# Eight sums of x per tile made by VectorE in place of GpSimd, in a three-layer float32 kernel on one Trainium2 core

## The reference

```python
def _moe_ref(x, w_in, w_out):
    h = x @ w_in                                  # 3072x512 by 512x2048
    g = np.where(h > 0.0, h, np.exp(np.minimum(h, 0.0)) - 1.0)
    return g @ w_out                              # 2048x512

def _moe2_ref(x, w_in, w_out, s, b):
    r = np.maximum(x @ w_in, 0.0)
    return (s * (r * r) + b) @ w_out
```

## Time and profile before

| | us |
|---|---|
| median of 3 runs | 1146.09 |
| lowest, highest | 1142.92, 1147.23 |
| the profiled execution | 1145.91 |
| its span in the profile | 1143.90 |
| PE busy | 1098.1 |
| DVE busy | 822.1 |
| ACT busy | 781.3 |
| POOL busy | 389.7 |

### The profile page before, as it was taken

The page is one execution under the profiler, slowest core; times in us unless marked ns, Lnnn a source line. Parts: engine busy times, 40 slices in busy tenths (PEclk is TensorE's granted clock), DMA queues, the critical chain, the costliest instruction groups (busy, mean ns, idle before and its releaser), DMA issues.

```text
span 1143.9 us, 18152 instructions
## 1 busy us (share of the span) xinstructions
PE 1098.1 (96%) x5787; PEld 876.1 (77%) x5787; DVE 822.1 (72%) x1210; ACT 781.3 (68%) x1842; POOL 389.7 (34%) x427
## 2 busy tenths in 40 slices
PE   8999898979999999989999999999999999999998
PEld 4667666757767778878788787888888888888886
DVE  5796686458886965898877968868848568576475
ACT  4797686667658757758758678667677476774574
POOL 5789689741232432136276113663000000000000
PEclk9999999989999999999999999999999999999999
DMA  9998999989889989869899789898697666776664
GB/s 202 268 273 254 345 330 354 348 268 323 251 237 251 269 256 263 280 210 348 301 358 348 233 263 373 300 349 282 186 282 233 189 198 189 219 218 193 194 192 158
DMA packets 204054, 302.80 MB, mean 265 GB/s; under 512 B 112824, under 2 KB 121016, under 8 KB 203960
## 3 DMA queue, kind: packets, MB, share of 16 engines
q1 hardware_dynamic: 203960, 301.65, 85.4%
HBM read 226.10 MB, written 75.50 MB: 264 GB/s over the span
## 4 chain that ended last, share of the span: by engine, by line
PE 73%; ACT 6%; DMA 6%; DVE 5%; issue 4%; POOL 3%; SPq 3%; ACTq 0%; POOLq 0%; DVEq 0%
PE ps L1020 35%; PE ps L1005 31%; DMA w_scratch<-w_new 3%; ACT ps L1100 2%; PE ps L914 2%; DMA w_ring<-w_scratch 1%; DVE g_lo L1494 1%; PE ps L939 1%; POOL w_new L801 1%; PE ps L966 1%; POOL att L801 1%; ACT elu L1193 1%; PE ps L923 1%; PE ps L908 1%; DVE nbias L1347 1%
## 5 line engine op out<-in xcount | busy, mean ns | idle before, releaser
L1005 PE MATMUL ps<-xc_hi,w_ring 128*128 128x512 f32 x1344 | 435.9, 397 | 5.0 <-ACT s L1166 3.7
L1020 PE MATMUL ps<-g_hi,w_ring 128*128 128x512 f32 x1344 | 420.4, 394 | 11.4 <-issue 6.4
L1005 PEld LDWEIGHTS ps<-xc_hi,w_ring 128*128 128x128 f32 x1344 | 253.9, 189 | 63.8 <-issue 4.0
L1020 PEld LDWEIGHTS ps<-g_hi,w_ring 128*128 128x128 f32 x1344 | 249.9, 189 | 68.3 <-issue 9.0
L1005 PE MATMUL ps<-xc_lo,w_ring 128*128 128x512 f32 x672 | 263.2, 392 | 0.0
L1020 PE MATMUL ps<-g_lo,w_ring 128*128 128x512 f32 x672 | 263.1, 392 | 0.0
L801 POOL TENSOR_TENSOR w_new<-w_raw,w_new 128x256 fp32r<-128x256 f32 x179 | 165.9, 933 | 219.0 <-ACT w_new L1247 215.8
L1494 DVE TENSOR_TENSOR g_lo<-X,g_hi 128x512 fp32r<-128x512 f32 x240 | 178.4, 748 | 30.5 <-ACT g_hi L1233 30.0
L1233 ACT ACTIVATE g_hi<-X 128x512 fp32r<-128x512 f32 x240 | 150.1, 629 | 56.8 <-PE ps L1020 55.1
L1020 PEld LDWEIGHTS ps<-g_lo,w_ring 128*128 128x128 f32 x672 | 126.7, 189 | 26.9
L1005 PEld LDWEIGHTS ps<-xc_lo,w_ring 128*128 128x128 f32 x672 | 127.2, 189 | 24.4
(11 more groups left out here) (125 smaller groups left out, 1350.5 us busy)
## 6 DMA issues: line engine op xcount, KB each, us to landing
w_ring<-w_scratch SPq DMA_DIRECT2D x336, 512.0 KB, 4.4
w_scratch<-w_new SPq DMA_DIRECT2D x179, 256.0 KB, 5.3
w_scratch<-att SPq DMA_DIRECT2D x45, 256.0 KB, 4.8
w_raw<-in_moe_w_in SPq DMA_DIRECT2D x16, 512.0 KB, 5.6
w_raw<-in_moe_w_out SPq DMA_DIRECT2D x16, 512.0 KB, 6.0
x_scratch<-y SPq DMA_DIRECT2D x12, 512.0 KB, 6.1
att<-x_scratch SPq DMA_DIRECT2D x12, 512.0 KB, 5.9
out<-elu SPq DMA_DIRECT2D x24, 256.0 KB, 4.3
```

The source lines that it names most:

```text
L1005: last = nc.tensor.matmul(bank_of(st, st.i), w[:, a, cols], x[:, st.pi, kk, :], start=(st.pi in (P1, P5) and kk == 0 and n == 0), stop=(kk ...
L1020: last = nc.tensor.matmul(bank_of(st, d), w[:, a, cols], x[:, k % RING, :], start=(st.pi in (P1, P5) + (P4,) * (1 - st.gr) and st.i == 0 a ...
```

## The change

POOL's `sums_of_x` and its two calls go. DVE gets `next_x_sum`, called in each step at the end of its list (before the copy of K^T), for the steps in the table `NEXT_SUMS`: P5 at 106 and 107, P6 at 108 and 109, P7 at 110 and 111, P4 at 114 and 115, each first kk = 0 and then kk = 1. Operands, results and shapes are unchanged; the count in `x_sum` follows the new order. The P4 sums lie in the next tile's steps 2 and 3.

```diff
+NEXT_SUMS = {106 + i: (pi, kk) for i, (pi, kk) in enumerate((pi, kk) for pi in (P5, P6, P7) for kk in range(2))}
+NEXT_SUMS.update({114: (P4, 0), 115: (P4, 1)})
...
         def x_sum(t, kk, pi):
             first = HEAD_SUMS + 8 * (t - 1)
-            return first + (7 + kk if pi == P4 else 3 * kk + {P5: 1, P6: 2, P7: 3}[pi])
+            return first + 2 * (P5, P6, P7, P4).index(pi) + kk + 1
...
-            def sums_of_x(t):
-                n = HEAD_SUMS + 8 * (t - 1)
-                for kk in range(2):
-                    pool.wait_ge(x_in[kk], 32 * t)
-                    x12, x22 = (x_from(t, kk, pi) for pi in (P7, P3))
-                    x11 = x_from(t, kk, P1)
-                    t2 = x_from(t, kk, P6)
-                    pool.wait_ge(x_lo_done, x_count(t) + x_index(t, kk, P1) + 1)
-                    nc.gpsimd.tensor_tensor(x11, x12, x11, ALU.subtract).then_inc(x_sums, 1)
-                    pool.wait_ge(x_sums, n + 3 * kk + 1)
-                    nc.gpsimd.tensor_tensor(t2, x22, x11, ALU.subtract).then_inc(x_sums, 1)
-                    nc.gpsimd.tensor_tensor(x12, x22, x12, ALU.subtract).then_inc(x_sums, 1)
-                for kk in range(2):
-                    x21, t2 = x_from(t, kk, P2), x_from(t, kk, P6)
-                    pool.wait_ge(x_lo_done, x_count(t) + x_index(t, kk, P6) + 1)
-                    nc.gpsimd.tensor_tensor(t2, x21, t2, ALU.subtract).then_inc(x_sums, 1)
...
             prepare(sets_of(PAIR))
-            sums_of_x(1)
             for m in range(SETS, SETS + 4):
                 prepare((m,))
-            sums_of_x(2)
             for m in range(SETS + 4, 2 * SETS):
                 prepare((m,))
...
+            def next_x_sum(t, kk, pi):
+                x11, x12, x21, x22 = (x_from(t, kk, b) for b in (P1, P7, P2, P3))
+                t2 = x_from(t, kk, P6)
+                if pi == P5:
+                    dve.wait_ge(x_in[kk], 32 * t)
+                    dve.wait_ge(x_lo_done, x_count(t) + x_index(t, kk, P1) + 1)
+                    to, a, b = x11, x12, x11
+                elif pi == P6:
+                    dve.wait_ge(x_sums, x_sum(t, kk, P5))
+                    to, a, b = t2, x22, x11
+                elif pi == P7:
+                    dve.wait_ge(x_sums, x_sum(t, kk, P5))
+                    to, a, b = x12, x22, x12
+                else:
+                    dve.wait_ge(x_lo_done, x_count(t) + x_index(t, kk, P6) + 1)
+                    to, a, b = t2, x21, t2
+                nc.vector.tensor_tensor(to, a, b, ALU.subtract).then_inc(x_sums, 1)
...
                 t, s = divmod(g, PER_TILE)
+                for xt in range(1, TPL):
+                    if g - PER_TILE * (xt - 1) in NEXT_SUMS:
+                        pi, kk = NEXT_SUMS[g - PER_TILE * (xt - 1)]
+                        next_x_sum(xt, kk, pi)
```

## The result

The changed kernel took 1139.11 us (median of 11 runs, 1133.73 to 1143.34), the kernel before 1145.78 (11 runs, 1142.57 to 1147.48): **ratio 0.9939, 95% interval 0.9922 to 0.9956**, or 7.0 us less (5.0 to 8.9). Forecast were 1139.8 us and a gain of 6.3.

What follows compares the result with a forecast made beforehand. PE was taken to bound the kernel, standing still where POOL's sums slow DVE at the ends of tiles one and two. 3.0 + 3.3 = 6.3 us off gave a median of 1139.8 us, range 1137.6 to 1143.8.

Steps and rivals of the forecast that it cites:

- What bounds: PE waits at the ends of tiles one and two: 6.8 us lost by start times, 5.7 shown as idle.
- End of tile one: Steps 107 to 112: 3.2 us lost, 3.0 without the switch of matmul kinds, all of it to come back.
- End of tile two: Steps 107 to 112: 3.8 us lost; DVE's operations replayed at 0.60 us leave 0.5 of new stall, 3.3 returned.
- A sum's price: Each new sum on DVE in steps 106 to 111: 0.60 us taken, bounds 0.60 without POOL and 1.70 with it.
- P4: Two sums on DVE in steps 114 and 115: cost 0, at worst 1.2 us lost a tile.
- ACT's wait: ACT's splits of x wait for DVE's sums instead of POOL's: cost 0; sums 2 us late would delay the seeds.
- POOL's order: First subtraction of the next weights can come up to 68 us earlier, the next POOL instruction waits for ACT: cost 0.
- The rule that the prediction set against the change: Two-input DVE work collides with POOL's SBUF reads; four P4 sums beside weight work could cost 4.4 us of DVE time.
- Given back: If DMA sets the time behind tile two's end, its gain is taken back: 3.0 us left, 1143.1 us; chance 0.17.
- More than the stages: Later waits of 0.72 us at 356.03 and 1.21 at 552.46 go too: 8.2 us gained, 1137.9; chance 0.08.
- DVE the bound: Slow rows aren't POOL's doing, sums cost 1.70 us each: some 9 us lost twice, 1164 us; chance 0.05.
- The change does what it says: Denies the rival that DVE stays at 1.7 us as weight work moves in: no change, 1146 us; chance 0.05.

Runs made afterwards that it cites:

- bunched: Changed kernel with three sums at step 106 and three at step 107 instead of one a step from 106 to 111; ratio 0.9973 to the kernel before.
- no_sums: Changed kernel with the eight sums of x for tiles two and three left out altogether; ratio 0.9913 to the kernel before.
- pool_reads: Changed kernel with six POOL subtractions a stage at the old place, reading a constant and writing a spare buffer; ratio 1.0022 to the kernel before.
- p4_pool: Changed kernel with the two P4 sums of a tile given back to POOL; ratio 0.9936 to the kernel before.
- pool_writes: Changed kernel with POOL writing zeros to a spare buffer 18 times a stage at the old place, reading nothing; ratio 0.9953 to the kernel before.
- doubled: Changed kernel with one more DVE subtraction of 128x512 behind each of the six sums of steps 106 to 111; ratio 1.0014 to the kernel before.

## Why the prediction was right, point by point

- **What bounds.** Two stages with PE waiting for a late g_lo: right. Taking the loss from start times gave 6.8 us, where idle time showed 5.7; what came back is 6.33 (6.05 in the stages and 0.28 in step 106), over the 5.2 that the idle view allowed and on the 6.3 taken from start times. That it falls on it is partly luck, as the next point says, and the 0.35 of steps 88 and 89 then goes off it.
- **End of tile one, 3.0 forecast: 2.66 measured from step 107 on, 2.94 with step 106.** Three errors nearly cancel. Starting the count at step 107 missed 0.28. The switch between kinds of matmul, put at 0.1 to 0.2, is 0.38, so only 2.79 could come back up to step 112 (11.55 - 8.76). And "so all of the 3.0 comes back" left out the wait by way of the maximum, which gave up 0.13 at step 115. Small here; bunched made it 1.2.
- **End of tile two, 3.8 less 0.5: 3.39 measured.** The replay put the g_lo of step 111 at 507.05 against step 108 at 503.57, 3.48 apart; they came at 502.40 and 498.95, 3.45 apart. The stalls at steps 111 and 114 were 0.1 each; with the slower matmuls right behind them they make 0.40, by no_sums (17.86 - 17.46).
- **A sum's price, 0.60 of 0.60 to 1.70:** right in every row of both stages. pool_reads shows what stands at the other end: beside POOL's weight subtraction the first sum takes 1.21.
- **Costs put at nothing.** P4: shown by p4_pool, for the stages. ACT's wait: no seed was late. POOL's order, "Cost 0": wrong by 0.35 us. The forecast saw that the weight subtraction would come earlier, but not what DVE does there; it fell on work for steps 88 and 89 of tile two. pool_writes shows that the same subtraction costs 0.5 us inside a stage. The rule that the prediction set against the change, from the Trainium skill ("SBUF — State Buffer", Who interferes with whom), thus holds in this trace, but not where the prediction feared it: the four P4 sums all take 0.68 us.
- **Rivals.** Given back: no (the load's wait did not grow), but for the 0.35. More than the stages: not found, and up to 1 us behind tile two can't be excluded. DVE the bound: not at 0.60, in doubled yes. The change does what it says.
- **Chances.** The gain of 7.0 us lies over the 5.7 us of half a per cent, but its interval begins at 5.0. The forecast gave "faster by over half a per cent" 0.56, and the runs leave about as much doubt.

## What to carry to other kernels

Work given to an idle engine isn't free if the two engines collide: look for rows of a busy engine that get longer exactly while the idle one works, and count what its operations cost the busy one (5.8 us for six) against what they would cost there (3.6). Then place them by what stands behind each in the engine's order, and follow every line to the engine that bounds: the late g_lo, but also the maximum, whose result comes back to PE by way of ACT and DVE. Look too at what stood behind the moved work on its old engine: it now starts earlier, and can collide elsewhere (0.35 us here). Where executions scatter by 5 to 10 us, a stage's length between two start times repeats to hundredths and tells apart what medians can't.

## What the runs showed of the hardware beyond what was expected

POOL's subtraction of 128x512 slows a two-input DVE row by 1.1 us when it reads two x blocks (rows 1.70 apart), by 0.85 when both inputs are the same 128x128 tile (1.45 apart), and 18 writes not at all. A single 128x256 subtraction by POOL cost one DVE row 0.46 to 0.53 us; in pool_writes PE lost the same, at step 88 of tile two 0.35. And the start of step 107 in tile one scatters over 4.9 us between executions. All of that arises ahead of step 80, as steps 80 to 105 repeat within 0.05 us; what makes the first 260 us vary wasn't tried and stays open.
